# The softmax denominators' inverse moves behind two row maxima, and its store behind the head's copies

## The reference

```
scores = scale * q @ k^T, masked where the hash buckets of q and k differ     (16 heads, 768 x 768)
attn   = exp(scores - rowmax) / (sum + 1e-9);  out = attn @ v                  (head_dim 64)
x      = out of the heads side by side                                         (1536 x 512)
x      = g(x @ w_in) @ w_out,  g(h) = h if h > 0 else exp(min(h,0)) - 1        (512 -> 2048 -> 512)
y      = x + gate * (relu(x @ w1[e]) @ w2[e]) for the tokens that are computed (8 experts of 1024)
```

## Time and profile before

| | us |
|---|---|
| median of three runs | 675.4 |
| the profiled execution, its own time | 674.42 |
| its span | 672.6 |
| TensorE busy | 640.5 (95%) |
| VectorE busy | 358.3 (53%) |
| ScalarE busy | 325.8 (48%) |
| GpSimd busy | 245.8 (37%) |
| granted TensorE clock, mean | 0.986 |

### The profile page before, as it was taken

One profiled execution on the slowest core, in us unless ns is written; L12 is line 12 of the kernel. 1 busy time (PEld: TensorE's weight loads), 2 busy tenths in 40 slices (PEclk: granted clock), 3 DMA queues, 4 the chain that ended last, 5 costly groups with the idle time before them and its releaser, 6 DMA issues.

```text
span 672.6 us, 9823 instructions
## 1 busy us (share of the span) xinstructions
PE 640.5 (95%) x3632; PEld 593.5 (88%) x3632; DVE 358.3 (53%) x495; ACT 325.8 (48%) x505; POOL 245.8 (37%) x206
## 2 busy tenths in 40 slices
PE   4799999999999999999999999999999968999996
PEld 3599999999999999999999999999999857999995
DVE  6888777778887752665232222222233357465551
ACT  2377777777777775655423332333333320443330
POOL 4145487777777789140300030000022008221111
PEclk9999999999999999999999999999999977999999
DMA  7663555766553404530100002000466772999000
GB/s 167 160 144 85 145 147 144 168 160 157 148 142 95 107 11 140 170 106 0 60 36 1 0 0 94 0 0 0 166 243 248 250 279 80 371 359 341 35 12 25
DMA packets 67960, 84.00 MB, mean 125 GB/s; under 512 B 34260, under 2 KB 44500, under 8 KB 67920
## 3 DMA queue, kind: packets, MB, share of 16 engines
q1 hardware_dynamic: 66640, 79.83, 39.9%
q0 software_dynamic: 1280, 3.65, 1.6%
HBM read 56.64 MB, written 8.44 MB: 97 GB/s over the span
## 4 chain that ended last, share of the span: by engine, by line
PE 91%; DMA 3%; DVE 2%; ACT 1%; issue 1%; SPq 1%; POOL 0%; POOLq 0%; ACTq 0%; DVEq 0%
PE banks L1244 20%; PE banks L1255 20%; PE banks L1368 9%; PE banks L1383 7%; PE banks L1208 5%; PE banks L1209 5%; PE banks L1210 5%; PE banks L1177 5%; PE banks L1192 5%; PE banks L1193 5%; PE banks L1161 2%; DMA y_rows<-y 2%; DVE row_max L846 1%; PE banks L1273 1%; PE banks L1168 1%
## 5 line engine op out<-in xcount | busy, mean ns | idle before, releaser
L1244 PE MATMUL banks<-x_hi,w_split 128*128 (+1 forms) x512 | 141.7, 337 | 0.0
L938 DVE SCALAR_TENSOR_TENSOR g<-exp_min_h,banks 128x384 f32<-128x384 f32 x64 | 35.4, 554 | 185.9 <-ACT exp_min_h L744 185.9
L515 POOL TENSOR_TENSOR probs_lo<-probs,probs_hi 128x768 fp32r<-128x768 f32 x64 | 108.0, 1705 | 55.7 <-ACT probs_hi L682 55.4
L1255 PE MATMUL banks<-w_split,g_hi 128*128 128x512 f32 x384 | 120.4, 394 | 0.1
L741 ACT ACTIVATE exp_min_h<-banks 128x384 f32<-128x384 f32 x64 | 31.5, 492 | 168.1 <-PE banks L1244 168.1
L674 ACT ACTIVATE probs<-banks 128x768 f32<-128x768 f32 x96 | 77.6, 808 | 57.2 <-PE banks L1193 57.0
L846 DVE TENSOR_REDUCE row_max<-banks 128x1 f32<-128x768 f32 x96 | 88.8, 954 | 27.9 <-PE banks L1177 27.8
L1244 PEld LDWEIGHTS banks<-x_hi,w_split 128*128 128x128 f32 x512 | 93.6, 188 | 2.7
L1244 PE MATMUL banks<-x_lo,w_split 128*128 (+1 forms) x256 | 86.0, 336 | 0.0
L1255 PEld LDWEIGHTS banks<-w_split,g_hi 128*128 128x128 f32 x384 | 70.6, 188 | 12.3 <-DVE g_lo L912 0.5
L682 ACT ACTIVATE probs_hi<-probs 128x768 fp32r<-128x768 f32 x96 | 80.7, 842 | 0.0
(11 more groups left out here) (163 smaller groups left out, 1035.8 us busy)
## 6 DMA issues: line engine op xcount, KB each, us to landing
expert_w<-in_moe_w SPq DMA_DIRECT2D x32, 1024.0 KB, 6.4
w_raw<-in_moe_w_in SPq DMA_DIRECT2D x16, 256.0 KB, 4.1
w_raw<-in_moe_w_out SPq DMA_DIRECT2D x16, 256.0 KB, 4.9
qk_nat<-in_q SPq DMA_DIRECT2D x16, 192.0 KB, 4.1
qk_nat<-in_k SPq DMA_DIRECT2D x16, 192.0 KB, 4.0
v_nat<-in_v SPq DMA_DIRECT2D x16, 192.0 KB, 4.0
q_hi_rows_T<-qk_hi_T SPq DMA_DIRECT2D x16, 192.0 KB, 3.1
k_hi_rows_T<-qk_hi_T SPq DMA_DIRECT2D x16, 192.0 KB, 3.4
```

What stands on the lines that cost most here:

```text
L515: pool.tensor_tensor(p_lo[:, n % RING, :, 0:HALF], probs[:, n % RING, :].rearrange("p (b n) -> p b n", b=2), p_hi[:, n % RING, :, 0:HALF]. ...
L1244: mm = pe.matmul(banks[:, j % 2, 0:BN], w, x, start=(c == 0 and w is hi and x is x_hi), stop=(c == KC - 1 and w is lo))
L1255: mm = pe.matmul(banks[:, 2 + t, :], g, W[:, j, part, :], start=(j == 0 and i == 0), stop=(j == FT - 1 and i == 2))
```

## The change

Two things move, nothing is added or removed.

- On SyncE, `store_rden` of odd heads from 3 on moves from before the v load and the six copies to after them, directly in front of `load_rden`.
- On VectorE, `inverse_den` of the same heads moves from before the first row maximum of the head to after the second (`t == 1`). In head 15 no row maximum is issued, and its order stays the same.

```diff
             for h in range(HEADS):
                 if h + 3 < HEADS:
                     load_qk(h + 3)
-                if h % 2 and h >= 3:
-                    store_rden(h // 2 - 1)
                 if h + 2 < HEADS:
                     load_v(h + 2)
                     copy_rows(h + 2)
                     copy_low_rows(h + 2)
                 if h % 2 and h >= 3:
+                    store_rden(h // 2 - 1)
                     load_rden(h // 2 - 1)
...
             for h in range(HEADS):
-                if h % 2 and h >= 3:
-                    inverse_den(h // 2 - 1)
                 for t in range(QT):
                     if h + 1 < HEADS:
                         maximum(h + 1, t)
                     if t == 0 and h + 2 < HEADS:
                         low_qk(h + 2)
+                    if t == 1 and h % 2 and h >= 3:
+                        inverse_den(h // 2 - 1)
```

## The result

The changed kernel takes 684.28 us (median of 4 runs, 683.06 to 687.35), the kernel before, in the same session, 674.96 (4 runs). The ratio is 1.0141, with a 95% interval of 1.0099 to 1.0182: slower, by about 9.3 us. The prediction was 676.0 with a range up to 681.0. The profiled execution took 682.89 us, with a span of 681.1 (before 674.42 and 672.6).

A forecast was written before the change was run, and what follows sets the result against it. TensorE's matmuls were taken to bound each head, with VectorE's series at its end. 0 (VectorE) + 0 (v, copies) + 0.6 (late `rden_rows`) on 674.4 us gave 675.0, as a median 676.0; range 673.8 to 681.0.

The forecast's parts named there:

- What bounds: Attention stage: a head costs TensorE's matmuls; VectorE's series at its end, with L853 stretched by GpSimd, adds small delays.
- VectorE's part at nothing: Moving the 0.23 us reciprocal behind two maxima in six heads costs and gains nothing; bounds 1.4 us either way.
- v and the copies at nothing: SyncE's queue in odd heads: the earlier v load is worth nothing, and the six copies keep their times.
- The store lands 3.8 us after its issue: SyncE's queue: the store lands 0.4 us behind the last copy, so `rden_rows` is issued 3.8 us later (2.4 to 4.2).
- `rden_rows` takes 10.0 us from issue to use: Load on two engines: 8.0 us of data plus 2.0 for start and landing; upper bound 10.7, from the last pair.
- One to one: End of even heads: lateness of `rden_rows` passes through L853 fully into the head; 1.05 us together, taken as +0.6.
- Turn-taking on the two engines: Open point: whether q, k, v and copies share `rden_rows`' two engines; set aside by ring order, otherwise nearer +6 us.
- the slower rival: Loads queued behind `rden_rows` take turns with it on its two engines, adding 1 to 2 us to the load.
- doubt about q's 6.9 us: q seemed to land before the 8 us load ahead; sharing one semaphore with k, it might be pieces of both.
- `normalise` starts late and holds VectorE: GpSimd in heads 4 to 14, once `rden_rows` lands late: +4.8 us, at worst +9.5 (684.9); chance 0.29.
- signs listed for "wrong": Even heads: L536 waits for `rden_rows`, L853 or VectorE's low parts over 0.6 us longer, heads over 15.2 us.
- "faster" case: The reciprocal's old place was in the chain, and late `normalise` clears L853: -2.6 us, 672.8; chance 0.06.

The follow-up runs named there:

- `after_spread`: The changed kernel with `rden_rows` loaded by two DMAs, one per head, each from one row to 64 partitions: 674.58 us, ratio 0.9995.
- `rden_alone`: The changed kernel with q and k issued ahead of `rden_rows`, and the next v load and copies held until it lands: 679.39 us, ratio 1.0047.
- `wait_only`: The changed kernel, GpSimd still waiting for `rden_rows` but skipping the product for the first six pairs: 1109.59 us on other values; head 8 takes 14.68 us.

## Why the prediction was wrong

- **What bounds.** Right. TensorE, with the end of each head as the tight place, and L853 as the coupling: the 6.93 us lost in heads 4 to 12 all stand in it or in the low parts behind it.
- **VectorE's part at nothing.** Right. The moved reciprocal takes 0.22 inside the maxima; the idle time before the next pair is 0.49, not the 0.33 forecast, because in the rows the reciprocal overlaps its neighbours (104.32 to 104.54, the next maximum from 104.46); the first maximum of an odd head has 0.73 of idle before it. `after_spread`, with both moves and a quick load, is at 0.9995.
- **v and the copies at nothing.** Right here: no wait of MAX for a copy in the changed kernel.
- **The store lands 3.8 us after its issue.** Right: 3.59 in head 7, and 3.52 to 3.59 in five heads, 4.50 in head 9, which the forecast had singled out.
- **`rden_rows` takes 10.0 us from issue to use. This is the step that failed.** It took 11.0 to 12.3, beyond the upper bound of 10.7 as well. In head 8 the sum was 5.95 (store, from head 7's first maximum) + 3.8 + 10.0 = 19.75 against 20.15 at which GpSimd is ready, 0.4 to spare; measured were 5.84 + 3.59 + 11.73 = 21.16 against 14.78 + 5.21 = 19.99, late by 1.17. Of that miss of 1.6 the load made 1.7 and the other terms -0.2. The same in each head turned "three pairs late, 1.05 us together" into five late, 6.6 us. The rate held (49 GB/s in quiet stretches again). The mis-sized term is the 2.0 for start and landing, taken from a small store, with nothing added for the copies that run beside the load's end; the bound, taken from a load with weights ahead of it, was too low as well. The packet records split head 7's load, 64 packets of 3 KB on each of the two engines: the first starts 1.35 us after the issue, the last is done 8.91 later, and GpSimd starts 1.47 after that. Left to itself a packet takes 0.12 us, 7.5 us for 64, so the 8.0 had half a microsecond too much in it; from 149.5 on, with the next head's copies under way, such packets take some 0.23. This load had no row with its own landing, and the sum had only 0.4 us of margin: a term read from another kind of transfer should have carried a microsecond or two of doubt by itself.
- **One to one.** Half right. Heads 4, 6, 10 and 12 gave 0.6 to 0.84 us per us of wait, head 8 gave 2.2. There the late product ended at 156.54, held the pad, and the fourth low part at 157.28 then met VectorE's second low part as well. The forecast bound of one GpSimd operation (1.9) was passed, at 2.52 there and 2.15 in head 10.
- **Turn-taking on the two engines.** The rule that the Trainium skill gives was used to set this aside, and the packets agree with it: in each pair 672 packets of q and 672 of k, fourteen sixteenths, ran early, and the 192 that belong to the two engines only behind `rden_rows`. What failed is the step from there to "nothing to add". From the load's last packet to GpSimd's start pass 1.4 to 1.5 us in the changed kernel, in the three pairs where both engines' ends can be told, and 0.5 to 0.7 to SyncE's next issue in `rden_alone`. So what is queued behind seems to cost its microsecond at the end of the load, by the copies that run beside it, and not by taking turns. The size of the slower rival, 1 to 2 us, was right; its mechanism wasn't. The prediction's doubt about q's 6.9 us fits as well: in the kernel before, the last packets of q and k ran from 145.33 to 146.85, and the landing of q at some 142.3 is where k's first fourteen sixteenths were done (142.02).
- **The rival was the case.** "`normalise` starts late and holds VectorE" had 0.29 and its worst sum, 684.9, is close to what came. That the number is so close is in part luck: the sum has 1.9 us in five heads, 9.5, and measured are 0.23 to 2.52, 6.9 together, with 1.6 us of the profiled span from elsewhere. The signs listed for "wrong" are all there: L535 waits for `rden_rows` in even heads, the pad and low parts run long, heads over 15.2 us in four of five. `wait_only` and `after_spread` together show the route.

## What to carry to other kernels

When a chain of store, load and use is moved to where nothing covers the store's flight, its slack is the difference of several times: write each with a row of its own kind, and don't call it even with 0.4 us left. Look first at how many DMA engines a broadcast load runs on: making its outermost dimension 64 instead of 2 took away the whole loss. And a wait on an engine off the critical path costs by what the operation behind it then collides with, so look at the neighbour's durations, not at the wait's.

## What the hardware showed that I hadn't expected

- The same load on two engines took 10.2 to 11.9 us with nothing issued behind it, 11.0 to 12.9 with v, copies or q and k behind; 7.5 of it is data at the bare 0.12 us per packet.
- With `rden_rows` on two engines, q and k behind it were done to fourteen sixteenths within 7 us of its issue, and had to wait for it with the rest. v, issued 5.6 us behind it in head 8, took 9.6 us to land; a head earlier, with no such load ahead, 3.3.
- GpSimd's and VectorE's operations on SBUF stretched each other by their overlap: the pad write from 0.17 to between 0.4 and 1.7 us, a pair of low parts from 1.81 to 3.50, GpSimd's `normalise` from 3.82 to 4.59, while the reciprocal stayed at 0.22. The Trainium skill ("SBUF — State Buffer", section "Who interferes with whom") says that a VectorE instruction with two SBUF inputs contends with a GpSimd one that reads SBUF, and one with a single input doesn't; the trace agrees in both.
- Shorter GpSimd operations were worth 0.6%, more than the 2.6 us of the prediction's "faster" case: three quarters of `normalise` end ahead of the pad write, and the fourth no longer meets it. The 672.5 to 673.5 that I had expected of it were too high by over a microsecond.
